# Linear attention and two expert layers: the decays multiplied in behind the transposes, the raw k and r transposed as they arrive

## The reference

```python
# r, k, v: (2, 8, 768, 48)   w, u: (8, 48)
for t in range(S):
    cur = einsum('bhd,bhe->bhde', u * k_t, v_t)          # the bonus of the present token
    y[t] = einsum('bhd,bhde->bhe', r_t, state + cur)
    state = w[:, :, None] * state + einsum('bhd,bhe->bhde', k_t, v_t)
x  = top-1 mixture of 8 experts (384 -> 1024 -> 384), all tokens kept
out = the same with other weights and a capacity for each expert
```

## Time and profile before

| what | us |
|---|---|
| median of 3 runs | 409.33 |
| lowest, highest | 407.27, 409.5 |
| the profiled execution | 410.13 |
| its span in the profile | 408.2 |
| PE, DVE, ACT, POOL busy in it | 355.6, 211.8, 138.4, 182.3 |

### The profile page before, as it was taken

How to read it: one execution, slowest core, us unless ns; L and a number is a source line. 1 busy time by engine, 2 the same in 40 slices (tenths; PEclk the granted TensorE clock), 3 DMA queues, 4 the chain that set the end, 5 groups by cost and what they waited for, 6 DMA issues and landing times.

```text
span 408.2 us, 10477 instructions
## 1 busy us (share of the span) xinstructions
PE 355.6 (87%) x3160; PEld 346.8 (85%) x3161; DVE 211.8 (52%) x539; ACT 138.4 (34%) x228; POOL 182.3 (45%) x304
## 2 busy tenths in 40 slices
PE   0699899934999999999999999148999999999990
PEld 0599899924999999999999998138999999999990
DVE  4368666687188855555555585193411454424310
ACT  1266455416255322222222242002522555345220
POOL 6797899705045633333333243142533443434411
PEclk9999999976799999999999999658999999999996
DMA  7999974142999211111111411108719999393100
GB/s 128 176 308 295 241 165 110 39 153 79 337 388 388 63 39 50 47 40 39 39 39 40 155 61 39 11 21 273 273 49 336 337 332 332 87 349 139 32 29 16
DMA packets 66650, 61.98 MB, mean 152 GB/s; under 512 B 43909, under 2 KB 59444, under 8 KB 66496
## 3 DMA queue, kind: packets, MB, share of 16 engines
q1 hardware_dynamic: 60800, 48.85, 38.0%
q0 software_dynamic: 3712, 10.22, 7.7%
q10 hardware_dynamic: 2112, 2.57, 2.0%
HBM read 52.85 MB, written 10.09 MB: 154 GB/s over the span
## 4 chain that ended last, share of the span: by engine, by line
PE 70%; POOL 8%; DVE 7%; issue 7%; DMA 4%; ACT 1%; POOLq 0%; ACTq 0%; DVEq 0%; SPq 0%
PE p_h L1142 37%; PE p_o L1164 28%; POOL sc L531 4%; PE p_xt L1120 3%; POOL prod L518 2%; DMA xg<-x_rows,src_idx 2%; POOL r_sc L513 1%; DMA w_col<-in_w 1%; DVE row_oh L348 1%; DMA lg<-x_rows 1%; DMA x_rows<-y_row,dst_now 1%; DVE k_sc L765 1%; POOL prod L520 1%; DVE st L783 1%; PE p_kt L1019 1%
## 5 line engine op out<-in xcount | busy, mean ns | idle before, releaser
L1142 PE MATMUL p_h<-xT,w_sb 128*128 128x128 f32 x1296 | 153.5, 280 | 1.4 <-ACT xT L628 1.4
L1142 PEld LDWEIGHTS p_h<-xT,w_sb 128*128 128x128 f32 x1296 | 152.6, 196 | 2.0 <-issue 2.0
L951 DVE SCALAR_TENSOR_TENSOR h_lo<-p_h,h_hi 128x512 fp32r<-128x512 f32 x54 | 37.3, 692 | 87.0 <-ACT h_hi L709 85.9
L968 DVE CUSTOM_DVE_ANT_0 lg_prod<-y_row,wg_all 128x384 f32<-128x384 f32 x112 | 55.7, 552 | 41.7 <-ACT y_row L719 41.5
L1164 PE MATMUL p_o<-w_hi,h_hi 128*128 x216 | 75.2, 348 | 0.0
L1164 PE MATMUL p_o<-w_lo,h_hi 128*128 x216 | 73.1, 339 | 0.0
L1164 PE MATMUL p_o<-w_hi,h_lo 128*128 x216 | 72.9, 338 | 0.0
L709 ACT ACTIVATE h_hi<-p_h 128x512 fp32r<-128x512 f32 x54 | 32.3, 598 | 115.5 <-PE p_h L1142 115.5
L543 POOL TENSOR_TENSOR dst_mark<-zeros 128x1 f32<-128x1 f32 x54 | 14.6, 271 | 106.8 <-DVE y_row L968 68.9
L797 DVE TENSOR_TENSOR w_lo<-w_raw,w_hi 128x1024 fp32r<-128x1024 f32 x36 | 43.7, 1265 | 8.3 <-ACT w_hi L628 8.3
L543 POOL TENSOR_TENSOR src_mark<-zeros 128x1 f32<-128x1 f32 x54 | 17.3, 321 | 54.1 <-PE p_xt L1120 34.3
(11 more groups left out here) (168 smaller groups left out, 390.6 us busy)
## 6 DMA issues: line engine op xcount, KB each, us to landing
w_raw<-in_moe_w SPq DMA_DIRECT2D x12, 1536.0 KB, 9.1
w_sb<-in_moe_w SPq DMA_DIRECT2D x12, 1536.0 KB, 9.3
k_raw<-in_k SPq DMA_DIRECT2D x12, 192.0 KB, 3.7
r_raw<-in_r SPq DMA_DIRECT2D x12, 192.0 KB, 3.7
v_raw<-in_v SPq DMA_DIRECT2D x12, 192.0 KB, 4.0
x_rows<-x_rows SPq DMA_DIRECT2D x12, 192.0 KB, 2.3
out<-zeros ACTq DMA_DIRECT2D x1, 2304.0 KB, 10.4
wg_nat<-in_moe_w_gate SPq DMA_DIRECT2D x1, 1536.0 KB, 6.3
```

Source lines behind the costliest of these rows:

```text
L951: stt(h_lo[:, at, :], p_h[n][:, :, :], 0.0, h_hi[:, at, :].bitcast(F32), ALU.max, ALU.subtract).then_inc(h_ready[layer], 1)
L968: last = nv.tensor_tensor_reduce(out=lg_prod[:, n, :], in0=y_row[par][:, 0:DM], in1=wg2_all[:, e, :], op0=ALU.mult, op1=ALU.add, scale=1.0 ...
L1142: last = mm(p_h[half][:, f, :], w1_sb[place][:, c, col:col + P], xT[:, c, :], start=(c == 0), stop=(c == DC - 1))
```

## The change

The raw k and r are transposed on PE as soon as they have landed, and are multiplied by the powers when they leave PSUM. So r_sc, r_tab and POOL's scaling of r go; kT and rT are now made by DVE (three multiplications out of PSUM, `turned`) and not by ACT; the scaled k, needed with tokens on the partitions for the state, is made by POOL, for n and not for n+1. The raw buffers of k and r have heads of 64 columns, 16 of them zero, so that they can be transposed in pairs. POOL makes half of sc's diagonal (j = 0) and ACT the other half with four copies (`diagonal`). k and r have semaphores apart from v's. The decays are loaded first on ACT's queue. The powers run to 64, the chunk's decay is the square of the last. PE does 18 warming matmuls before the first turn and 12 each before and behind the turn of the powers. `values` no longer waits for rT and yT, which its predecessors in PE's stream have waited for.

```diff
-                for to, src in ((k_raw[q][:, :, :], k_t), (r_raw[q][:, :, :], r_t), (heads(v_raw[q]), v_t)):
+                for to, src, done in ((k_raw[q][:, :, 0:D], k_t, kr_loaded), (r_raw[q][:, :, 0:D], r_t, kr_loaded),
+                                      (heads(v_raw[q]), v_t, v_loaded)):
                     sp.dma_start(to, src[b, bass.ds(c, 1), :, :, :].rearrange("n t h d -> (n t) h d"))\
-                        .then_inc(raw_loaded[q], 16)
+                        .then_inc(done[q], 16)
...
-            sp.wait_ge(ones_set, 1)
-            with nc.allow_non_contiguous_dma(reason="a few hundred decays, one to a partition"):
-                for j in range(2):
-                    sp.dma_start(w_col[HD * j:HD * j + D, :], w_jd[j]).then_inc(w_loaded, 16)
...
+            gp.memset(w_col[:, :], 1.0).then_inc(ones_set, 1)
+            for t in r_raw:
+                last = gp.memset(t[:, :, D:HD], 0.0)
+            last.then_inc(pads_clear, 1)
...
-            def scale_r(i, q, n, b):
-                pool.wait_ge(raw_loaded[q], 48 * (i + 1))
-                wait_pos(pool, kr_turned, n - 1)
-                gp.tensor_tensor(r_sc[b][:, :, :, 0:D], by_head(r_raw[q]), r_tab[:, :, :, 0:D], ALU.mult)\
-                    .then_inc(r_scaled, 1)
             def unit(i, q, n, b, c):
+                pool.wait_ge(kr_loaded[q], 32 * (i + 1))
                 wait_pos(pool, bonus_sum, n)
-                gp.tensor_tensor(prod1[:, :, :], r_raw[q][:, :, :], u_tab[:, :, :], ALU.mult).then_inc(bonus_prod, 1)
+                gp.tensor_tensor(prod1[:, :, :], r_raw[q][:, :, 0:D], u_tab[:, :, :], ALU.mult).then_inc(bonus_prod, 1)
                 pool.wait_ge(bonus_prod, 2 * n + 1)
-                gp.tensor_tensor(prod2[:, :, :], prod1[:, :, :], k_raw[q][:, :, :], ALU.mult).then_inc(bonus_prod, 1)
-                if q < RING - 1:
-                    scale_r(i, q + 1, n + 1, 1 - b)
-                else:
-                    if isinstance(i, int):
-                        scale_r(i + 1, 0, n + 1, 1 - b)
-                    else:
-                        with pool.If(i < NU // RING - 1):
-                            scale_r(i + 1, 0, n + 1, 1 - b)
+                gp.tensor_tensor(prod2[:, :, :], prod1[:, :, :], k_raw[q][:, :, 0:D], ALU.mult).then_inc(bonus_prod, 1)
+                if isinstance(n, int) and n == 0:
+                    pool.wait_ge(tables_ready, 1)
+                wait_pos(pool, kv_made, n - 1)
+                gp.tensor_tensor(k_sc[b][:, :, 0:D], k_raw[q][:, :, 0:D], k_tab[:, :, 0:D], ALU.mult).then_inc(k_scaled, 1)
                 pool.wait_ge(bonus_sum, n + 1)
                 wait_pos(pool, y_made, n - 1)
-                gp.tensor_tensor(sc[b][:, :, :, :], ident[:, :].unsqueeze(1).unsqueeze(2).broadcast_to([P, 2, HP, T]),
-                                 bonus[:, :].rearrange("p (g j) -> p j g", j=2).unsqueeze(3).broadcast_to([P, 2, HP, T]),
+                gp.tensor_tensor(sc[b][:, 0, :, :], ident[:, :].unsqueeze(1).broadcast_to([P, HP, T]),
+                                 bonus[:, :].rearrange("p (g j) -> p j g", j=2)[:, 0, :].unsqueeze(2).broadcast_to([P, HP, T]),
                                  ALU.mult).then_inc(bonus_diag, 1)
-            pool.wait_ge(tables_ready, 2)
-            scale_r(0, 0, 0, 0)
             units(pool, unit)
...
+            act.wait_ge(ones_set, 1)
+            with nc.allow_non_contiguous_dma(reason="a few hundred decays, one to a partition"):
+                for j in range(2):
+                    act.dma_start(w_col[HD * j:HD * j + D, :], w_jd[j]).then_inc(w_loaded, 16)
+            act.dma_start(u_tab[:, :, :], u.partition_broadcast(P)).then_inc(small_in, 16)
...
+            act.wait_ge(powers_turned, 1)
+            copy(k_tab[:, :, :].rearrange("p (g j) d -> p g (j d)", j=2)[:, :, 0:R], p_x[:, :, 0:R]).then_inc(tables_ready, 1)
+            act.wait_ge(consts, 1)
...
+            def diagonal(n, b):
+                act.wait_ge(bonus_sum, n + 1)
+                wait_pos(act, y_made, n - 1)
+                for g in range(HP):
+                    last = sa.activation(sc[b][:, 1, g, :], ident[:, :], ACT.Copy, scale=bonus[:, 2 * g + 1:2 * g + 2])
+                last.then_inc(bonus_diag, 1)
             def unit(i, q, n, b, c):
-                act.wait_ge(kr_turned, n + 1)
-                wait_pos(act, scored, n)
-                copy(kT[0:R, :, :], p_kt[0:R, :, :]).then_inc(kT_ready, 1)
-                wait_pos(act, y_made, n - 1)
-                for j in range(2):
-                    at = slice(HD * j, HD * j + D)
-                    last = copy(rT[b][at, j, :, :], p_rt[at, :, :])
-                last.then_inc(rT_ready, 1)
+                diagonal(n, b)
...
+            for t in rT:
+                nv.memset(t[:, :, :, :], 0.0)
+            nv.memset(kT[:, :, :], 0.0).then_inc(cleared, 1)
...
-            ch.do(nv.reciprocal(pinv[:, :, :], pw[:, :, 0:T // 2 + 1]))
-            M = T // 2
             nv.tensor_copy(pk[:, :, 0:M], pw[:, :, M - 1::-1])
-            nv.tensor_copy(pk[:, :, M:T], pinv[:, :, 1:M + 1]).then_inc(powers_ready, 1)
-            nv.tensor_copy(pr[:, :, 0:M], pinv[:, :, M:0:-1])
+            ch.do(nv.reciprocal(pk[:, :, M:T], pw[:, :, 1:M + 1]))
             nv.tensor_copy(pr[:, :, M:T], pw[:, :, 0:M]).then_inc(powers_ready, 1)
-            pairs = lambda t: t[:, :, :].rearrange("p (g j) d -> p g j d", j=2)
-            decay = pw[:, :, T:T + 1].broadcast_to([P, HP, D])
+            nv.tensor_copy(pr[:, :, 0:M], pk[:, :, T - 1:M - 1:-1]).then_inc(powers_ready, 1)
+            tt(decay[:, :], pw[:, :, M], pw[:, :, M], ALU.mult)
+            dve.wait_ge(powers_ready, 2)
...
-            def scale_k(i, q, n, b):
-                dve.wait_ge(raw_loaded[q], 48 * (i + 1))
-                wait_pos(dve, kv_made, n - 1)
-                tt(k_sc[b][:, :, :, 0:D], pairs(k_raw[q]), k_tab[:, :, :, 0:D], ALU.mult).then_inc(k_scaled, 1)
+            def turned(n, b):
+                dve.wait_ge(kr_turned, n + 1)
+                wait_pos(dve, scored, n)
+                tt(kT[0:R, :, :], p_kt[0:R, :, :], pk[0:R, :, :], ALU.mult).then_inc(kT_ready, 1)
+                wait_pos(dve, y_made, n - 1)
+                for j in range(2):
+                    at = slice(HD * j, HD * j + D)
+                    last = tt(rT[b][at, j, :, :], p_rt[at, :, :], pr[at, :, :], ALU.mult)
+                last.then_inc(rT_ready, 1)
...
+                turned(n, b)
...
+            def keep_clock(at, count):
+                for n in range(count):
+                    mm(at[:, 0:P], ones_b[:, :], before_b[:, :], start=(n == 0), stop=(n == count - 1))
+            pe.wait_ge(consts, 2)
+            keep_clock(p_y[:, 0, :], WARM_SETUP)
+            pe.wait_ge(pads_clear, 2)
+            def turn_powers():
+                pe.wait_ge(powers_ready, 1)
                 for g in range(HP):
-                    last = turn(p_t[:, g, 0:R], t[0:R, g, :], ident[0:R, 0:R])
+                    last = turn(p_x[:, g, 0:R], pk[0:R, g, :], ident[0:R, 0:R])
                 last.then_inc(powers_turned, 1)
-            pe.wait_ge(tables_ready, 2)
-            pe.wait_ge(cleared, 3)
-            pe.wait_ge(small_in, 16 * N_SMALL)
-            def turn_kr(n, b):
-                pe.wait_ge(k_scaled, n + 1)
+                pe.wait_ge(cleared, 3)
+                pe.wait_ge(small_in, 16 * N_SMALL)
+            def turn_kr(i, q, n):
+                pe.wait_ge(kr_loaded[q], 32 * (i + 1))
                 wait_pos(pe, kT_ready, n)
                 for g in range(HP):
-                    turn(p_kt[0:R, g, :], two(k_sc[b], g), ident[:, :])
-                pe.wait_ge(r_scaled, n + 1)
+                    turn(p_kt[0:R, g, :], two(k_raw[q], g), ident[:, :])
                 wait_pos(pe, rT_ready, n)
                 for g in range(HP):
-                    last = turn(p_rt[0:R, g, :], two(r_sc[b], g), ident[:, :])
+                    last = turn(p_rt[0:R, g, :], two(r_raw[q], g), ident[:, :])
...
+                pe.wait_ge(k_scaled, n + 1)
+                pe.wait_ge(v_loaded[q], 16 * (i + 1))
...
+                turn_kr(i, q, n)
+                if isinstance(n, int) and n == 0:
+                    keep_clock(p_y[:, 0, :], WARM_TURN)
...
```

89 lines of the change are left out of this document (33 added, 56 removed).

## The result

| | before | after |
|---|---|---|
| median of the runs, us | 408.95 (407.27 to 412.66, 6 runs) | 413.18 (411.52 to 414.85, 6 runs) |
| span of the profiled execution, us | 408.2 | 410.8 |
| mean granted TensorE clock | 0.945 | 0.945 |
| M(0), first masking copy | 18.91 | 12.99 |
| M(11), last masking copy | 80.58 | 84.42 |

What follows compares the result with a forecast made beforehand. PE and POOL were taken to compete for the loop's bound, behind a serial start. Start 13.1 plus steps 68.42 gave last mask 81.5, 0.9 later: 410.13 + 0.9 = 411.1 us (median 410.3), own range 408.0 to 412.5, wide 405.0 to 414.5.

Steps and rivals of the forecast that it cites:

- rival A: Loop: DVE's decay is not stretched, 0.28 in place of 0.84, so PE's 5.36 rules; 405.1 us; chance 0.22.
- Rival B: Loop, slower: ACT's four diagonal copies take 1.66 us, deciding from 1.1 on; 416.8 us; chance 0.15.
- The start: Ahead of the loop: the first masking copy comes at 13.1 us, 5.8 us earlier.
- The evictions: Loop, DVE: kT and two rT multiplications out of PSUM take 0.62 + 0.69 + 0.69 = 2.00 us, unstretched.
- Rival D: Start: decays land late behind k and r, first mask near 14.6; 411.8 us; chance 0.57 together with the forecast.
- The ring: Loop: mask, decay, evictions, bonus, half diagonal and handovers in a closed round, 5.86 us a unit, replacing PE's 5.36.
- Rival C: Loop, slower: POOL stretches evictions out of PSUM, about 1 us a unit; 420 us or more; chance 0.06.
- the wait for w_raw: Unit 1: ACT waits for w_raw, landing at 22.6, before splitting it; 0.9 us lost once (0 to 1.2).
- w_lo: Units 2 and 3: DVE's splitting of w2, behind the decay and ahead of the evictions, costs 1.95 us twice.
- Cost nothing: Loop: loads go out some 2 us later but land over 5 us before their turn, so no cost.
- On a path that PE had already overtaken: Loop: POOL's given-up r scaling and half diagonal, 2.2 us, lay off the bound, taken as PE's 5.36.
- The sum: First mask 13.1 plus 68.42 for eleven steps puts the last mask at 81.5, 0.9 us later than before.

Runs made afterwards that it cites:

- Decay first: The changed kernel with the state's decay on DVE in front of the masking copy, not behind it; ratio to before 0.9986 [0.9951, 1.0020].
- late split: The changed kernel with ACT splitting w2's first part in unit 2, the others in unit 3, and DVE both low parts in unit 3; ratio to before 1.0071.
- late split with zeros and w1 late: The late split, plus output zeros issued behind the first layer's experts and the first expert's w1 behind SP's loop; ratio to before 1.0019 [0.9997, 1.0042].
- orders only: The changed kernel with late split, decay before the masking copy, and ACT's rows and logits before its diagonal, transfers unchanged; ratio to before 0.9971 [0.9940, 1.0002].

## Why the prediction was right in its sign and short in its size

- **Where the time fell.** The profiled execution took 412.56 for 411.1, and the median was 413.18 for 410.3. That is outside the forecast's own range of 408.0 to 412.5, and inside the wide one, 405.0 to 414.5, which also made room for the rivals A and B; neither of them is why it landed there.
- **The start was right, with some luck.** M(0) 12.99 for 13.1; the decays there at 5.38 for 5.5, the reciprocal 1.74 for 1.76. The evictions began 0.5 before their forecast (8.76 for 9.25) and the bonus was there at 11.40 for 11.8, but from there to the mask it took 1.59 in place of 1.3, with ACT's copies at 1.28. That DVE can be held beside POOL's first product, as in six of the later profiles (M(0) up to 13.80), has no term in the sum. Rival D did not come about.
- **The ring was right.** 5.87 for 5.86. Within it the decay costs 0.66 in place of 0.84. It is still held until POOL's product ends (55.80 + 1.00 = 56.80; decay to 57.01), but it starts later against it. ACT's four copies take 1.28 in place of 1.1 and end 0.20 behind POOL's half, so that the diagonal with its handover takes 1.42 in place of 1.18. That the sum is right to 0.01 is luck: the decay's -0.18 and the diagonal's +0.24 cancel, with -0.05 in the small terms. Decay first confirms the ring by breaking it, and is rival A's pace, 5.36, by an edit: in the changed kernel itself the decay stood on the ring, and A did not come.
- **The evictions were right**, at 0.60 + 0.69 + 0.69 and the bonus 0.03 behind. The Trainium skill (VectorE: DVE Perf Modes, "Two Vector instructions with no wait between them") says that an instruction on another quarter of the partitions is held until those before are finished. The rows now agree on DVE: kT to rT 0.60 at a duration of 0.68, two rT 1.38 and no overlap behind them. Rival C's stretching of PSUM operations beside POOL did not show: kT, at 56.94, takes 0.68 although all of it lies beside POOL's k scaling, which runs from 56.76 for 1.13.
- **Rival B** had the mechanism, ACT's copies deciding, but not its price: 0.30 to the next and 0.39 for the last, where B had 0.39 and 0.49. The 1.28 is beyond B's 1.1 by 0.18.
- **The step that failed is the wait for w_raw**: "1.5 us earlier now, landing at 22.6 … 0.9 lost once (0 to 1.2)". It was issued at 17.73, not near 15.5. SP's loads began 1.5 earlier (0.82), but the next issue behind them came at 14.19, and in before at 14.36; then the four small issues took 3.54 in place of 2.65. So the first issue does not set when the last one leaves. That the pace of the transfers does is the reading that fits, not one that a run tested. w_raw took 8.63 in place of 7.1 and landed at 26.36. The 3.76 later landing is the whole difference of the step: 6.76 + 3.76 = 10.52, measured 10.53. The end of this wait is bound to the absolute time of a transfer, while everything around it had been moved 5.8 earlier; I had moved the transfer 1.5 earlier, with SP's first issue, where it came 0.7 later. What the wait cost in the end is less than its size: late split takes it away and is no faster, since the next wait stands behind it, on which the forecast had no cost.
- **The second misjudged term is w_lo**, 1.95 twice. Both took about 1.2, since POOL was between two operations each time. In step 2→3 PE's slow groups took the place of what was saved: the scores ended at 36.44, and mask 3 followed them and not the diagonal (7.75 for 7.81, right by luck). In 3→4 nothing did, 6.94 for 7.81. Where POOL does run, the held price is real, 3.21 for two.
- **"Cost nothing" for the loads** was right in the changed kernel only because w_raw's wait covered it: late split uncovers it at unit 5, with a step of 10.69.
- **"On a path that PE had already overtaken"** was too strong for what POOL gave up: POOL's round of 5.30 paced the masks of before, with PE's 5.36 just behind. The sum is not hurt by it, since it has the ring's 5.86 over both.
- **The sum.** M(11) 84.42 for 81.5: +3.01 in the steps (71.43 - 68.42; 3.77 of it in step 1→2, -0.87 in 3→4), -0.11 at the start. Of the 3.84 against before, 2.6 are left in the span, and the medians differ by 4.2, 413.18 for 410.3 forecast.

## What to carry to other kernels

When the start of a loop is moved earlier, mark every wait in it that ends by the clock of a transfer and not by the work around it, and leave it where it was: the loop's first units then pay the difference. Before you call one such wait the cause, ask what stands late behind it; here two in series hid each other, and only removing both brought mask 5 forward. When an engine gives up work so that two others halve it, write out the ring through all three, since its sum (5.87) can exceed the busy time of each.

## What the runs showed of the hardware that I had not expected

- The twelve loads keep SP issuing from 0.82 to 14.19 us in after, and from 2.33 to 14.36 in before. Starting 1.5 earlier lets the issue behind them go 0.2 earlier.
- Behind 5.27 us of idle time (granted clock 0.88 from 23 to 29 us, then 0.50 from 29 to 34), groups of matmuls take 2.06, 1.94 and 1.10 where they took 1.15, 1.06 and 0.67: the lower of TensorE's two levels, 1.2 GHz, by that clock and by their durations. It costs about 2.2 us of PE time in one unit.
- DVE's w_lo takes 1.22 with POOL idle, and 2.07 for the first of two beside POOL's scaling of k (3.21 for the pair, in the late split with zeros and w1 late), while kT from PSUM takes 0.68 beside the same operation. A plain copy is held too: the last copy of the powers takes 0.28 in after and 1.10 beside POOL's first product in orders only.
- With the zeros moved late, ACT's y rows wait for DMA five times in the first layer's part, 18.7 us in sum. With w1 late too the last mask is at 80.67 and the span 408.4, as in before (80.58 and 408.2), so no cost of this wait shows at the end.
